# Logits of a mixture's last two tiles placed by one-hot matrix products, and first rows transposed ahead of the schedule

## The reference: what is computed

```
q, k, v: (4, 8, 576, 64)
out = softmax(q_c @ k_c.T / 8) @ v_c            # in each chunk of 64 rows
x   = out as (N, D) = (2304, 512)

# first mixture (E = 8 experts, F = 1024)
logits = x @ w_gate                              # (N, E)
e = argmax(logits); gate = softmax(logits)[e]
eom = sigmoid(x @ w_output_gate)
x = gate * eom[e] * (relu(x @ w1[e]) @ w2[e])

# second mixture: the same with its own weights, no output gate;
# in token order, an expert keeps its first 576 tokens, the others give zero
logits = x @ w_gate
...
out = gate * (relu(x @ w1[e]) @ w2[e])
```

## Time and profile before

| | us |
|---|---|
| median of 3 runs | 706.04 (705.34 to 706.71) |
| the profiled execution, its own time | 706.62 |
| its span, first to last instruction | 704.9 |
| TensorE busy | 605.6 (86%) |
| DVE busy | 448.7 (64%) |
| GpSimd busy | 406.4 (58%) |
| ScalarE busy | 185.6 (26%) |
| mean granted TensorE clock | 0.933 of 2.4 GHz |

### The profile page before, as it was taken

One profiled execution on the slowest core, in us unless ns is written; L12 is line 12 of the kernel. 1 busy time (PEld: TensorE's weight loads), 2 busy tenths in 40 slices (PEclk: granted clock), 3 DMA queues, 4 the chain that ended last, 5 costly groups with the idle time before them and its releaser, 6 DMA issues.

```text
span 704.9 us, 14919 instructions
## 1 busy us (share of the span) xinstructions
PE 605.6 (86%) x4106; PEld 492.3 (70%) x4107; DVE 448.7 (64%) x1037; ACT 185.6 (26%) x241; POOL 406.4 (58%) x276
## 2 busy tenths in 40 slices
PE   4887873899999999999996139999999999999573
PEld 3766652688888888888884037888888888887462
DVE  3887757469879999889997574354543545433340
ACT  2678742022240222423321200022023200244110
POOL 1146313394797649799987210663667671779760
PEclk9999985899999999999998658999999999999796
DMA  9899860487465326566666101523434541346600
GB/s 210 215 286 282 238 214 15 166 315 265 153 224 189 120 106 216 168 202 226 199 203 207 27 17 30 166 96 105 156 128 166 174 163 46 132 160 210 221 23 16
DMA packets 79308, 113.75 MB, mean 161 GB/s; under 512 B 27737, under 2 KB 46169, under 8 KB 79152
## 3 DMA queue, kind: packets, MB, share of 16 engines
q1 hardware_dynamic: 67616, 86.00, 39.8%
q0 software_dynamic: 8000, 25.17, 10.5%
q10 hardware_dynamic: 3664, 2.20, 1.0%
HBM read 94.57 MB, written 20.00 MB: 163 GB/s over the span
## 4 chain that ended last, share of the span: by engine, by line
PE 72%; DVE 9%; issue 6%; DMA 5%; ACT 3%; POOL 2%; POOLq 1%; ACTq 1%; DVEq 0%; SPq 0%
PE b L1043 20%; PE b L1045 19%; PE b L1044 19%; PE b L1065 4%; PE b L1038 2%; POOL wl L438 2%; PE b L965 2%; DMA ring<-in_moe_w 2%; PE b L943 2%; PE b L953 1%; ACT wh L619 1%; DMA x<-y,sidx 1%; DMA out<-y,sidx 1%; DVE kT L684 1%; DMA cap_i<-in_capacity 1%
## 5 line engine op out<-in xcount | busy, mean ns | idle before, releaser
L438 POOL TENSOR_TENSOR wl<-ring,wh (+1 forms) x128 | 302.8, 2393 | 31.5 <-ACT wh L619 26.8
L619 ACT CAST wh<-ring 128x1024 f32 (+1 forms) x112 | 113.0, 1048 | 398.2 <-PE b L1045 314.4
L1043 PE MATMUL b<-wh,hTh 128*128 x320 | 132.5, 414 | 11.7 <-DVE hTl L857 11.7
L1043 PE MATMUL b<-wh,xTh 128*128 x320 | 131.4, 411 | 5.5 <-DVE xTl L844 3.7
L1044 PE MATMUL b<-wh,hTl 128*128 x320 | 128.7, 402 | 0.0
L1045 PE MATMUL b<-wl,hTh 128*128 x320 | 128.6, 402 | 0.0
L1045 PE MATMUL b<-wl,xTh 128*128 x320 | 127.9, 400 | 0.0
L1044 PE MATMUL b<-wh,xTl 128*128 x320 | 127.6, 399 | 0.0
L880 DVE SCALAR_TENSOR_TENSOR unread<-b,gates,wg_rows 128x512 f32<-128x512 f32 x160 | 110.1, 745 | 1.2 <-PE b L1045 1.2
L829 DVE TENSOR_SCALAR h<-b 128x512 f32<-128x512 f32 x80 | 55.5, 696 | 55.6 <-PE b L1045 54.1
L866 DVE CAST sidx<-b 128x1 int32 (+1 forms) x40 | 6.6, 164 | 129.2 <-PE b L1045 67.3
(11 more groups left out here) (147 smaller groups left out, 640.2 us busy)
## 6 DMA issues: line engine op xcount, KB each, us to landing
ring<-in_moe_w SPq DMA_DIRECT2D x128, 512.0 KB, 3.3
vin<-in_v SPq DMA_DIRECT2D x72, 64.0 KB, 4.3
x<-xrow POOLq DMA_DIRECT2D x18, 256.0 KB, 5.6
out<-zeros SPq DMA_DIRECT2D x18, 256.0 KB, 3.5
qin<-in_q SPq DMA_DIRECT2D x6, 512.0 KB, 6.9
kin<-in_k SPq DMA_DIRECT2D x6, 512.0 KB, 6.0
wg_rows<-in_moe_w_gate ACTq DMA_DIRECT2D x1, 2048.0 KB, 7.1
qin<-in_q SPq DMA_DIRECT2D x2, 384.0 KB, 5.7
```

What stands on the lines that cost most here:

```text
L438: nc.gpsimd.tensor_tensor(low, src, high.bitcast(F32), ALU.subtract).then_inc(wl_here, 1)
L619: nc.scalar.copy(dst, ring[:, i % RING]).then_inc(wh_here, 1)
L1043: nc.tensor.matmul(dst, high, weights(wh, *wt), start=start, stop=False)
```

## The change

Three things.

1. **Logits of the last two tiles.** ScalarE no longer loads `logits` after the last scatter, but after the one of the third-last tile (`most_logits`, in the middle of the second expert's rounding of mixture two). The logit columns of x2 are zeroed at the start of the kernel, so that the rows of the last two tiles read as zero. The scatters of these two tiles wait until that load is done (`lg2_in`). Their logits are added from the chip instead: for each row of the tile, `late_places` works out from its token number which token tile and which position it is, as two one-hot tables, by comparison with the numbers 0 to 127, which lie in PSUM (`ps_numbers`); `late_logits` multiplies the tile table with the eight logits; and TensorE's product of the position table with that puts each logit into its place in `ps_late`. DVE adds it to `logits` before lmax.
2. **The ends of the streams.** GpSimd's scatter of the third-last tile stands ahead of the last step's weight parts. The last tile's `scaled` stands in DVE's second routing, between upto and count (`last_rows`), and its scatter in GpSimd's second routing; the first gather of mixture two waits for that scatter. `sidx` is now made by a maximum with zero.
3. **First rows.** `rows_T(0)` of each mixture stands ahead of TensorE's wait for `routed` and of the loads of its table values.

```diff
+        ps_late = b23[:, 0:NT * E]
+        ps_numbers = b7[:, 0:P]
...
# GpSimd
                 pool.sem_inc(gsum_ready, 1)
+                if m == 1:
+                    scatter(total - 1)
                 pool.wait_ge(gate_whole, m + 1)
...
+                    pool.wait_ge(lg2_zero, 16)
                 pool.wait_ge(index_ready, m + 1)
+                if m == 1:
+                    pool.wait_ge(y_out[0], total * 16)
                 gather_first(0)
...
-                def step(g, ahead=True):
+                def step(g, ahead=True, first=False):
                     lo, middle, hi = due(m, g)
+                    if first:
+                        scatter(g - behind)
                     split(lo, middle)
-                    if reached(g, behind):
+                    if reached(g, behind) and not first:
                         scatter(g - behind)
...
-                step(total - 1, ahead=False)
+                step(total - 1, ahead=False, first=(m == 0))
                 if m == 0:
+                    pool.wait_ge(lg2_in, 16)
                     scatter(total - 2)
-                scatter(total - 1)
-                if m == 0:
-                    pool.wait_ge(y_out[m], total * 16)
-                    stand_alone(pool)
+                if m == 1:
+                    scatter(total - 1)
# ScalarE
+            act.wait_ge(s_const, 1)
+            act.dma_start(x2[:, D:ROW].rearrange("(t p) e -> p t e", p=P),
+                          zeros[:, 0:NT * E].rearrange("p (t e) -> p t e", e=E),
+                          allow_slow_non_contiguous=True).then_inc(lg2_zero, 16)
...
-            round_expert(1, 1, (0, total))
-
-            act.wait_ge(y_out[0], total * 16)
-            act.dma_start(logits[:, :, 0:E], x2[:, D:ROW].rearrange("(t p) e -> p t e", p=P),
-                          allow_slow_non_contiguous=True).then_inc(lg2_in, 16)
+            def most_logits():
+                act.wait_ge(y_out[0], (total - 2) * 16)
+                act.dma_start(logits[:, :, 0:E], x2[:, D:ROW].rearrange("(t p) e -> p t e", p=P),
+                              allow_slow_non_contiguous=True).then_inc(lg2_in, 16)
+            round_expert(1, 1, (0, total), most_logits)
# DVE, routing
+                if m == 1:
+                    dve.wait_ge(late_done, 1)
+                    link(nc.vector.tensor_tensor(lg, lg, ps_late.rearrange("p (t e) -> p t e", e=E), ALU.add))
                 nc.vector.tensor_reduce(lmax[:, :], lg, AX.X, ALU.max).then_inc(top_ready, 1)
...
                                              0.0, ALU.mult, ALU.add).then_inc(upto_ready, 1)
+                if m == 1:
+                    last_rows()
                 dve.wait_ge(rank_done, m + 1)
# DVE, body
-                    nc.vector.tensor_copy(sidx[:, :], at(ps_scatter, j))
+                    nc.vector.tensor_scalar_max(sidx[:, :], at(ps_scatter, j), 0.0)
...
+                def late_link(instruction):
+                    late_steps[0] += 1
+                    instruction.then_inc(late_step, 1)
+                    dve.wait_ge(late_step, late_steps[0])
+
+                def late_places(k, j):
+                    late_link(nc.vector.tensor_scalar(late_w[:, k, 0:1], at(ps_scatter, j), 1.0 / P, -63.75 / P, ALU.mult, ALU.add))
+                    late_link(nc.vector.tensor_scalar(late_w[:, k, 1:2], late_w[:, k, 0:1], ROUND, -ROUND, ALU.add, ALU.add))
+                    late_link(nc.vector.scalar_tensor_tensor(out=late_w[:, k, 2:3], in0=late_w[:, k, 1:2], scalar=-float(P),
+                                                             in1=at(ps_scatter, j), op0=ALU.mult, op1=ALU.add))
+                    nc.vector.tensor_scalar(late_pos[:, k, :], ps_numbers, late_w[:, k, 2:3], None, ALU.is_equal)
+                    late_link(nc.vector.tensor_scalar(late_tile[:, k, :], ps_numbers[:, 0:NT], late_w[:, k, 1:2], None, ALU.is_equal))
+
+                def late_logits(k, j):
+                    dve.wait_ge(next_lg_here, (j + 1) * E)
+                    nc.vector.tensor_tensor(late_lg[:, k, :, :], late_tile[:, k, :].unsqueeze(2).to_broadcast([P, NT, E]),
+                                            next_lg.unsqueeze(1).to_broadcast([P, NT, E]), ALU.mult).then_inc(late_ready, 1)
...
                         x_split(1)
+                        if m == 0:
+                            late_link(nc.vector.tensor_copy(ps_numbers, iota_i[:, :]))
                         return
...
+                    if tail and m == 0:
+                        late_places(0, g - 1)
+                        late_places(1, g)
                     if m == 0 and reached(g, 1):
                         next_logits(g - 1, range(E // 2, E))
+                        if tail:
+                            late_logits(0, g - 1)
                         scaled(g - 1)
...
                     if m == 0 and tail:
                         next_logits(g, range(E))
-                    if m == 1 or tail:
+                        late_logits(1, g)
+                    if m == 1:
                         scaled(g)
                 expert_steps(dve, m, step)
+                if m == 0:
+                    last_rows = functools.partial(scaled, tiles_of(dve, 0) - 1)
# TensorE
-                pe.wait_ge(routed, m + 1)
...
                     if head:
-                        rows_T(0)
                         first, before = expert_of(0)
...
+                rows_T(0)
+                pe.wait_ge(routed, m + 1)
                 expert_steps(pe, m, step)
+                if m == 0:
+                    for k in range(2):
+                        pe.wait_ge(late_ready, k + 1)
+                        last = nc.tensor.matmul(ps_late, late_pos[:, k, :], late_lg[:, k, :, :].rearrange("p t e -> p (t e)"),
+                                                start=(k == 0), stop=(k == 1))
+                    last.then_inc(late_done, 1)
```

More of the change, by code:

```diff
@@ L1 @@
+import functools
 from contextlib import ExitStack
@@ L89, in build @@
         pick = sb("pick", [P, 2 * E])
-        lgT = sb("lgT", [P, P])
         logits = sb("logits", [P, NT, 2 * E])
@@ L147, in build @@
             xrow = early("xrow", [P, XS, G, 2, DH])
+            lgT = early("lgT", [P, P])
         with ExitStack() as routing:
@@ L172, in build @@
         unread = sb("unread", [P, 2, D])
+        late_w = sb("late_w", [P, 2, 3])
+        late_tile = sb("late_tile", [P, 2, NT])
+        late_pos = sb("late_pos", [P, 2, P])
+        late_lg = sb("late_lg", [P, 2, NT, E])
         wg2_rows = sb("wg2_rows", [P, E, D])
@@ L197, in build @@
         wg2_in = sem("wg2_in")
+        lg2_zero = sem("lg2_zero")
+        late_step = sem("late_step")
+        late_ready = sem("late_ready")
+        late_done = sem("late_done")
         next_lg_here = sem("next_lg_here")
@@ L524, in gather, with scatter @@
                                                  bounds_check=N - 1, oob_is_err=False).then_inc(g_in[m], 16)
-                def scatter(g):
+                def scatter(g, m=m, dst=dst, width=width):
                     pool.wait_ge(y_here[m], g + 2)
@@ L605, in _, with round_expert @@
                     round_first(t - LAG)
-            def round_expert(m, e, used):
+            def round_expert(m, e, used, between=None):
                 mixture, last = used
                 for i in range(PX):
+                    if i == PW and between:
+                        between()
                     if i == 0:
@@ L859, in hidden_low, with scaled @@
                         ALU.subtract).then_inc((hT0_here, hT1_here)[half][m], 1)
-                def scaled(j):
+                def scaled(j, m=m):
                     dve.wait_ge(y_done[m], j + 1)
@@ L871, in scaled @@
                                             ALU.mult).then_inc(y_here[m], 1)
+                late_steps = [0]
+                def late_link(instruction):
[13 more added lines that the diff above has]
+                                            next_lg.unsqueeze(1).to_broadcast([P, NT, E]), ALU.mult).then_inc(late_ready, 1)
                 def next_logits(j, experts):
```

## The result

The changed kernel takes 697.75 us (median of 4 runs, 697.22 to 699.20), the kernel before 705.69 beside it (4 runs): ratio 0.9895, interval 0.9876 to 0.9914. That is 7.9 us less, with an interval of 6.1 to 8.8; a second comparison, beside later experiments, gave 697.87 against 704.64, ratio 0.9891 (0.9870 to 0.9913), 6.8 us less. By the ratios, which are not those of the two medians, the gains are 7.4 and 7.7 us. The forecast was 6.45 us less, the range 698.0 to 702.6 for a median of 706.04; beside 705.69 that range begins at 697.65, so the result lies at its lower edge.

The account below looks back on a forecast made before the run. TensorE's matrix products bound the kernel, with latency in the gap between mixtures. The sum -4.55 + 0.55 - 1.25 - 1.4 + 0.2 = -6.45 us takes the median 706.04 to 699.6 us; range 698.0 to 702.6.

Parts of the forecast that it names:

- The gap is latency, and two transfers in series are what can leave it: Between the mixtures TensorE idles 14.8 us; taking the last scatter and logits load off the chain gains 4.55 us.
- c's logits: Gate logits of mixture one's last tile, on DVE: begin 0.95 us later, at 390.4 instead of 389.43.
- From c's logits to lmax: End of mixture one: last tile's gate logits begin at 390.4, routing's first step at 397.8 instead of 402.35.
- The signs it named: Right: lmax 8.6 us after the last product, logits load landed before 389; wrong: a late_places step over 0.3 us.
- c's rows in the routing: Scaling the last tile's rows between upto and count on DVE costs 0.55 us (0.45 to 0.9).
- First rows ahead: At each mixture's head, transposing the first rows before the schedule ends gains 1.4 us in mixture one, 1.25 in two.
- a's scatter first, at no cost: Third-last tile's scatter ahead of GpSimd's weight parts: DVE's wait for it disappears; the delayed parts cost nothing.
- Rival 3: Between the mixtures, a late scatter of the last or second-last tile costs up to 4 us, 703.6; chance 5%.
- Rival 1: End of mixture one: DVE's rounding steps wait for GpSimd's running part, up to 4.6 us, 704.2 at most; chance 12%.
- sharing costs a tenth of a microsecond: DVE's two-input SBUF product took 0.31 us with GpSimd idle, 0.39 beside it; no wait for the other's instruction.
- Rival 4: Zeroing x2's logit columns delays attention's loads and makes the kernel slower: median 708.2 at 60 ns a packet; chance 3%.
- the 0.2 us: Cost assumed for zeroing x2's logit columns beside attention's first loads, out of 0 to 1.3 us.

Follow-up runs that it names:

- placing_only: Changed kernel with the first rows turned behind the wait for the schedule again: 701.62 us, ratio 0.9955 to the kernel before.
- rows_only: Kernel before with only the first rows turned ahead of the wait for the schedule: 703.06 us, ratio 0.9983 to the kernel before.
- parts_first: Changed kernel with GpSimd's weight parts again ahead of the third-last tile's scatter in mixture one's last step: 698.75 us, ratio 0.9924 to the kernel before.
- late_scatter: Changed kernel with the last tile's scatter issued on GpSimd after the gate's parts, not before the wait for the gate: 702.26 us, one run.
- zero8: Changed kernel with seven more zeroings of the same shape, to a scratch tensor, on ScalarE's queue at the start: 713.83 us, ratio 1.0111 to the kernel before.

## Why the prediction was right, and what it missed

- *The gap is latency, and two transfers in series are what can leave it.* Shown by placing_only: the column from c's last product to lmax falls from 21.05 to 16.64, **4.41 us against 4.55**. The mechanism is right. The closeness leans on the profile of before that the forecast was read from: against rows_only the same column gives 4.84, since the old wait moves with the clock of c's last product and the new one does not. Inside the 4.41 two terms were off and nearly cancel. The two late_places took 2.45 us and not 2.2 (the 128-number comparison 0.35, with longer gaps at its links), and c's logits begin 1.3 us and not 0.95 later, counted from the start of c's last product. From c's logits to lmax it is 7.2 us and not 7.4: the addition took 0.34, not 0.45, and the one-hot product 1.01 from table to addition, 1.05 forecast.
- *The signs it named:* the logits load is down at 383.8, no DMA piece stands in the chain between the mixtures, and xTh follows the end of the schedule by 0.80 and 0.69 us, close to the 0.7 written. Two signs came out against it. lmax follows the end of c's last product (385.99) by 9.4 us and not 8.6, because DVE is now the late one and this product was shorter (6.81 us for 7.48). And a late_places step took 0.35 us, where one longer than 0.3 was to count as wrong; it was not held, it is only dearer than the 0.26 in the sum.
- *c's rows in the routing:* 0.52 us against 0.55.
- *First rows ahead:* 1.28 and 1.24 against 1.4 and 1.25; rows_only shows them alone. The gathers land before the schedule's end, as the earlier trace rows said.
- *a's scatter first, at no cost:* no cost is seen in the columns, and no use either (parts_first); the times leave about 1 us open.
- *Rival 3, the new wait:* its mechanism exists and its price is 3.4 us once the cover is gone (late_scatter). The cover was read rightly: c's scatter is down at 402.4, the gather issued at 408.2. With b's scatter down at 392.0 and wanted at 397.7, that one had cover too.
- *Rival 1, GpSimd holds DVE:* the step that the earlier trace rows "speak against it" was wrong, and so was the sentence that sharing costs a tenth of a microsecond. SBUF-to-SBUF comparisons of 18 and 128 numbers are held until the last of the parts in a row has ended. The forecast held because the tables read PSUM, and because the one SBUF-to-SBUF step has a single number. The rows I leaned on were two-input products beside GpSimd instructions of 0.2 to 0.7 us, with gaps between them; they say little of a single-input one beside 9.4 us without a gap. The Trainium skill (VectorE: DVE Perf Modes, Why PSUM operands drop a tier) says the two-port mode needs both SBUF read ports, so a PSUM operand excludes it; with the sharing rule cited in the prediction that fits this case's traces, where a 128-number comparison took 0.35 us from PSUM beside the parts and 5.75 from SBUF. These two passages do not say why the single number was not held.
- *Rival 4, the zeroing writes:* the 0.2 us is not confirmed. It is below what these runs can tell, and zero8 measured something else, ScalarE's issuing. The sum for this rival counts the 0.2 twice: 60 ns a packet would make 708.0 and not 708.2.
- *The measured 7.9 against 6.4:* the edit's own columns give 6.41, or 6.84 with rows_only's wait. The second comparison gave 6.8 by the medians, 7.7 by its ratio. The rest is not explained by a mechanism; the variation of attention and of the bodies is larger than it. That the columns come within 0.04 us of the sum of 6.45 is in part luck: the terms that they show were forecast 0.24 us too high together, and the 0.2 for the zeroing, which they do not hold, makes up for it.

## What to carry to other kernels

Cut the profiles of all variants at the same events. Short stretches that one engine sets by itself repeat to hundredths and tell an edit of 1 us where the timed medians, with an attention stage that moves by several, cannot. A stretch that ends with a TensorE product after a gap does not: it moves with the number of instructions at half clock, so look at the product's length before you take a difference. When a table is made on VectorE beside long GpSimd work, let it read PSUM, or make it where GpSimd is idle: SBUF to SBUF it cost the whole gain here. A small computation that depends only on a schedule belongs where the engine waits anyway. What its removal from the end then gives is set by whatever comes last in its place, here TensorE's last product.

## What the runs showed of the hardware that I had not expected

- A VectorE comparison from SBUF to SBUF, of 18 or 128 numbers per partition, waited 5.2 to 5.5 us until a row of four GpSimd subtractions (9.4 us, no gaps) had ended, and not only until the running one had; one of a single number took 0.15 us beside them. GpSimd was not slowed.
- ScalarE's queue took 0.5 us to issue the first transfer of 2304 pieces of 32 bytes and 18.4 us for the next seven, 1.0 to 3.9 each on the chain; the DMA engines were 90% busy or more for most of that time, and whether that is the cause was not tried.
- Attention and the routing behind it ended anywhere from 119.9 to 125.1 us in thirteen profiles, with the same code up to there but for the one zeroing.
- The 24 instructions of one product took 6.81 to 8.09 us from first to last issue in kernels with the same code for it, with 7 to 13 of the steps at half-clock pace.
